# Gated net's spatial and output weights: loaded whole over their own low parts and split within the token mixer's last batch

## What is computed

```python
# 1: gated linear attention, 8 heads of 48, state over t
state = f[:, :, t, :, None] * state + einsum('bhd,bhe->bhde', k[:, :, t], v[:, :, t])
y[:, :, t] = einsum('bhd,bhde->bhe', q[:, :, t], state)
# 2: token mixer
theta = x @ w_theta
zr, zi = x * cos(theta), x * sin(theta)
u = x + einsum('ts,bsd->btd', w_tok_r, zr) + einsum('ts,bsd->btd', w_tok_i, zi)
x2 = u + maximum(u @ w_ch, 0)
# 3: gated net, d_ff = 1024, halves of 512
h = maximum(x2 @ w_in, 0);  u, v = halves of h
v_n = (v - mean(v)) / sqrt(var(v) + 1e-6)
v_s = einsum('ts,bsd->btd', w_spatial, v_n) + b_spatial
out = (u * v_s) @ w_out
```

## Time and profile before

| | us |
|---|---|
| Median of 3 runs | 621.71 (621.22 to 622.42) |
| The profiled execution, its own time | 619.17 |
| Its span, first to last instruction | 617.2 |
| PE busy | 580.9 (94%) |
| DVE busy | 367.0 (59%) |
| ACT busy | 290.6 (47%) |
| POOL busy | 34.7 (6%) |
| Share of DMA queue q1 in 16 engines' span | 31.4% |

### The profile page before, as it was taken

The page is one execution under the profiler, slowest core; times in us unless marked ns, Lnnn a source line. Parts: engine busy times, 40 slices in busy tenths (PEclk is TensorE's granted clock), DMA queues, the critical chain, the costliest instruction groups (busy, mean ns, idle before and its releaser), DMA issues.

```text
span 617.2 us, 11905 instructions
## 1 busy us (share of the span) xinstructions
PE 580.9 (94%) x4226; PEld 559.9 (91%) x4226; DVE 367.0 (59%) x614; ACT 290.6 (47%) x509; POOL 34.7 (6%) x66
## 2 busy tenths in 40 slices
PE   0999998789999999999999999899999999999998
PEld 0888887689999999999999998898999899989997
DVE  7899998466776538454955557557145713571151
ACT  5799996765553335242644225415331533153112
POOL 3232332000000000000000000000000000000000
PEclk9999999879999999999999999899999999999999
DMA  7879999262410231022013243500040001000102
GB/s 187 201 228 246 267 252 314 59 219 93 192 38 27 65 102 39 25 76 89 0 43 115 76 144 109 207 2 1 25 129 2 0 25 51 0 1 27 52 0 78
DMA packets 31546, 58.76 MB, mean 95 GB/s; under 512 B 3728, under 2 KB 23184, under 8 KB 31504
## 3 DMA queue, kind: packets, MB, share of 16 engines
q1 hardware_dynamic: 31504, 58.21, 31.4%
HBM read 44.04 MB, written 14.16 MB: 94 GB/s over the span
## 4 chain that ended last, share of the span: by engine, by line
PE 72%; DVE 3%; issue 3%; ACT 1%; DMA 1%; DVEq 0%; ACTq 0%; SPq 0%
PE mix_ps L1054 24%; PE gate_ps L1054 16%; PE ringc L1054 10%; PE theta_bank L1054 10%; PE small_ps L1054 10%; PE small_ps L1436 1%; DVE stats L1998 1%; DVE w_lo L78 1%; DMA wc_stage<-in_wC_dram 1%; ACT w_hi L73 0%; ACT v L1848 0%; DVE vn L2016 0%; DVE ang L1574 0%; DVE ang L1571 0%; DVE z L1590 0%
## 5 line engine op out<-in xcount | busy, mean ns | idle before, releaser
L1054 PE MATMUL mix_ps<-w_lo,z_hi 128*128 128x384 f32 x288 | 97.3, 338 | 2.0 <-issue 2.0
L1054 PE MATMUL mix_ps<-w_hi,z_hi 128*128 128x384 f32 x288 | 99.0, 344 | 0.0
L1054 PE MATMUL mix_ps<-w_hi,z_lo 128*128 128x384 f32 x288 | 97.6, 339 | 0.0
L1054 PE MATMUL gate_ps<-w_hi 128*128 128x384 f32 x192 | 64.9, 338 | 4.1 <-issue 4.1
L1054 PE MATMUL gate_ps<-w_hi,w_lo 128*128 128x384 f32 x192 | 64.7, 337 | 0.0
L1054 PE MATMUL gate_ps<-w_lo,w_hi 128*128 128x384 f32 x192 | 64.7, 337 | 0.0
L1054 PEld LDWEIGHTS mix_ps<-w_hi,z_lo 128*128 128x128 f32 x288 | 54.6, 190 | 2.2 <-issue 2.2
L1054 PEld LDWEIGHTS mix_ps<-w_lo,z_hi 128*128 128x128 f32 x288 | 54.6, 190 | 0.0
L1054 PEld LDWEIGHTS mix_ps<-w_hi,z_hi 128*128 128x128 f32 x288 | 54.6, 189 | 0.0
L73 ACT ACTIVATE g_hi<-gate 128x384 fp32r<-128x384 f32 x32 | 16.8, 526 | 78.6 <-DVE gate L2048 78.6
L2044 DVE TENSOR_TENSOR gate<-gate_ps,b_all 128x384 f32<-128x384 f32 x32 | 17.8, 557 | 59.7 <-PE gate_ps L1054 59.5
(11 more groups left out here) (163 smaller groups left out, 1417.1 us busy)
## 6 DMA issues: line engine op xcount, KB each, us to landing
f_raw<-in_fT_dram SPq DMA_DIRECT2D x32, 144.0 KB, 3.9
k_raw<-in_kT_dram SPq DMA_DIRECT2D x32, 144.0 KB, 3.3
q_raw<-in_qT_dram SPq DMA_DIRECT2D x32, 144.0 KB, 3.8
v_raw<-in_vC_dram SPq DMA_DIRECT2D x16, 288.0 KB, 4.0
xT<-y_sb SPq DMA_DIRECT2D x32, 144.0 KB, 3.7
xt<-xT SPq DMA_DIRECT2D x8, 576.0 KB, 4.0
w_raw<-in_wB_dram SPq DMA_DIRECT2D x6, 768.0 KB, 6.7
u<-xT SPq DMA_DIRECT2D x8, 576.0 KB, 5.0
```

The costliest lines, as they stand in the source:

```text
L1054: done = pe.matmul(out, a, b, start=(first and n == 0), stop=(last and n == len(terms) - 1))
```

## The change

`wc_stage` and the staged loads are taken out. `SpatialWeights` holds the new semaphores. SP's `load_w_c` issues, in the mixer's round 4 and for batch 3, three loads of 2048 columns (1 MB each) from wC into the first 6144 columns of `w_raw`, that is, into the place of the low parts; it waits until PE has used the token weights of s = 0 to 3 of the last batch (`mix_used` at 4). ACT's `w_c_up(0)` to `(5)` stand in round 5 behind `u_up(1)`. DVE's `w_c_down(0)` to `(3)` stand between the additions of round 5, and the low parts 4 and 5 are split in the gated net at the two places where parts 0 and 1 were (`w_down(4)`, `w_down(5)`); the four later splits of DVE and all of ACT's are gone from the gated net. PE's program is the same.

```diff
--- before
+++ after
+WC_LOADS = 3
...
+class SpatialWeights:
+    def __init__(self, nc, ctx, w_hi, w_lo, w_raw):
+        self.w_hi, self.w_lo, self.w_raw = w_hi, w_lo, w_raw
+        self.raw_in = [ctx.enter_context(nc.semaphore(f"c_raw_in{i}")) for i in range(WC_LOADS)]
+        self.hi_done = ctx.enter_context(nc.semaphore("c_whi_done"))
+        self.lo_done = ctx.enter_context(nc.semaphore("c_wlo_done"))
+
+    def up(self, act, n):
+        cols = slice(n * PART, (n + 1) * PART)
+        act.wait_ge(self.raw_in[n * WC_LOADS // WC_PARTS], 16)
+        split_hi(act, self.w_hi[:, cols], self.w_raw[:, cols]).then_inc(self.hi_done, 1)
+
+    def down(self, dve, n):
+        cols = slice(n * PART, (n + 1) * PART)
+        dve.wait_ge(self.hi_done, n + 1)
+        split_lo(dve, self.w_lo[:, cols], self.w_raw[:, cols], self.w_hi[:, cols]).then_inc(self.lo_done, 1)
+
+    def wait_for(self, eng, cols):
+        eng.wait_ge(self.hi_done, -(-cols // PART))
+        eng.wait_ge(self.lo_done, -(-cols // PART))
...
@@ token_mix, sync
+            def load_w_c(b):
+                if last_batch(b):
+                    sp.wait_ge(mix_used.h, mix_used.at(b, 4))
+                    for i in range(WC_LOADS):
+                        at, n = i * WC_COLS // WC_LOADS, WC_COLS // WC_LOADS
+                        sp.dma_start(part(w_raw, at, n), part(wC, W_IN_COLS + at, n)).then_inc(spatial.raw_in[i], 16)
...
-                        + [(load_residual, 1), (load_w_in, 1)], 2, 1)
+                        + [(load_residual, 1), (load_w_in, 1), (load_w_c, 1)], 2, 1)
...
@@ token_mix, scalar
+            def w_c_up(n):
+                def f(b):
+                    if last_batch(b):
+                        spatial.up(act, n)
+                return f
...
-                    (z_up(1), 1), (to_turns(2), 1), (u_up(0), 2), (u_up(1), 2), (trigs(2), 1), (xn_out(3), 1), (weights_up(2), 1), (w_in_up(0), 1),
+                    (z_up(1), 1), (to_turns(2), 1), (u_up(0), 2), (u_up(1), 2)] + [(w_c_up(n), 2) for n in range(WC_PARTS)] + [(trigs(2), 1), (xn_out(3), 1), (weights_up(2), 1), (w_in_up(0), 1),
...
@@ token_mix, vector (w_c_down(n) calls spatial.down(dve, n) for the last batch)
-                    (z_down(2), 1), (reduce(3), 1), (add_channel(0), 2), (multiply(3), 1), (add_channel(1), 2),
+                    (z_down(2), 1), (reduce(3), 1), (add_channel(0), 2), (multiply(3), 1), (add_channel(1), 2), (w_c_down(0), 2),
...
@@ gated_net, sync
-            for n in range(WC_PARTS):
-                if n >= STAGES:
-                    sp.wait_ge(whi_done, n - STAGES + 1)
-                    sp.wait_ge(wlo_done, n - STAGES + 1)
-                sp.dma_start(stage[n % STAGES][:, :], part(wC, W_IN_COLS + n * PART, PART)).then_inc(w_in[n % STAGES], 16)
...
@@ gated_net, scalar
-            def w_up(n):
-                def f(b):
-                    if first(b):
-                        act.wait_ge(w_in[n % STAGES], 16 * (n // STAGES + 1))
-                        split_hi(act, part(w_hi, n * PART, PART), stage[n % STAGES][:, :]).then_inc(whi_done, 1)
-                return f
...
@@ gated_net, vector
-                        dve.wait_ge(whi_done, n + 1)
-                        split_lo(dve, part(w_lo, n * PART, PART), stage[n % STAGES][:, :], part(w_hi, n * PART, PART))\
-                            .then_inc(wlo_done, 1)
+                        spatial_weights.down(dve, n)
...
-                (moments(2), 1), (normalise(1), 1), (vn_down(0), 1), (w_down(0), 1),
+                (moments(2), 1), (normalise(1), 1), (vn_down(0), 1), (w_down(4), 1),
...
-                (moments(4), 1), (normalise(3), 1), (vn_down(2), 1), (w_down(1), 1),
+                (moments(4), 1), (normalise(3), 1), (vn_down(2), 1), (w_down(5), 1),
...
-                (w_down(2), 1), (w_down(3), 1), (w_down(4), 1), (x_lo, 0), (w_down(5), 1), (gates, 1)], 2)
+                (x_lo, 0), (gates, 1)], 2)
```

More of the change, by code:

```diff
@@ L1090, in v_group, with token_mix @@
             both(in_hi, in_lo, k * DFF + FH, FH)) for k in range(DT)]).then_inc(gates.v_ps.h, 1)
-def token_mix(nc, sems, gates, waits_passed, w_hi, w_lo, w_raw, wb_hi, wb_lo, wB, wC, in_hi, in_lo, in_raw, xt, xt_hi, xt_lo,
+class SpatialWeights:
[15 more added lines that the diff above has]
+        eng.wait_ge(self.lo_done, -(-cols // PART))
+def token_mix(nc, sems, gates, spatial, waits_passed, w_hi, w_lo, w_raw, wb_hi, wb_lo, wB, wC, in_hi, in_lo, in_raw, xt, xt_hi, xt_lo,
               xn, mixing, rest, ident, half_pi, xT, x2T):
@@ L1660, in add_channel, with w_c_down, f @@
                 return f
+            def w_c_down(n):
+                def f(b):
+                    if last_batch(b):
+                        spatial.down(dve, n)
+                return f
             def first_x():
@@ L1711, in token_mix, with gated_net @@
                 "const_ready": const_ready, "x2_done": x2_done, "x2_out": x2_out}
-def gated_net(nc, sems, block, gates, mixer, waits_passed, w_hi, w_lo, in_hi, in_lo, xt, xt_hi, xt_lo, eps, early, late, stage, wC, bias,
+def gated_net(nc, sems, block, gates, spatial_weights, mixer, waits_passed, w_hi, w_lo, in_hi, in_lo, xt, xt_hi, xt_lo, eps, early, late, bias,
               x2T, out):
@@ L1785, in weights_ready @@
             if first(b):
-                eng.wait_ge(whi_done, -(-cols // PART))
-                eng.wait_ge(wlo_done, -(-cols // PART))
+                spatial_weights.wait_for(eng, cols)
         @block.sync
@@ L2114, in attention_and_mixers @@
         tail_lo = Region(nc, w_lo_at + 4 * EARLY_COLS)
-        STAGE_AT = VN_AT + ST * FH
-        stage = [t for at in (w_hi_at, w_lo_at) for t in Region(nc, at + 4 * STAGE_AT).take(f"wc_stage{at}_", [128, PART])]
         flag_ready = sems.enter_context(nc.semaphore("flag_ready"))
@@ L2122, in attention_and_mixers @@
         theta_in = sems.enter_context(nc.semaphore("theta_in"))
+        spatial = SpatialWeights(nc, sems, w_hi, w_lo, w_raw)
         with ExitStack() as banks:
             gates = Gates(nc, sems, [banks.enter_context(nc.psum_tensor(name, [128, 512], F32)) for name in ("theta_bank", "small_ps")])
-            mixer = token_mix(nc, sems, gates, waits_passed, w_hi, w_lo, w_raw, wb_hi, wb_lo, wB, wC, in_hi, in_lo, in_raw,
+            mixer = token_mix(nc, sems, gates, spatial, waits_passed, w_hi, w_lo, w_raw, wb_hi, wb_lo, wB, wC, in_hi, in_lo, in_raw,
                               xt, xt_hi, xt_lo, xn, mixing, rest, ident, half_pi, x_by_batch, x2T)
@@ L2153, in attention_and_mixers @@
                 banks.enter_context(nc.psum_tensor(f"mixer_bank{_}", [128, 512], F32))
-            gated_net(nc, sems, block, gates, mixer, waits_passed, w_hi, w_lo, in_hi, in_lo, xt, xt_hi, xt_lo, eps, early, late, stage,
-                      wC, bias, x2T, out)
+            gated_net(nc, sems, block, gates, spatial, mixer, waits_passed, w_hi, w_lo, in_hi, in_lo, xt, xt_hi, xt_lo, eps, early, late,
+                      bias, x2T, out)
 _INS = ["qT", "kT", "fT", "vC", "wB", "wC", "bias"]
```

18 lines of the change are left out of this document (7 added, 11 removed).

## The result

| | before | after |
|---|---|---|
| Median, us | 621.47 (620.64 to 622.42, 4 runs) | 613.91 (613.55 to 615.63, 4 runs) |
| Profiled execution, own time, us | 619.17 | 613.82 |
| Its span, us | 617.2 | 611.9 |
| PE busy, us | 580.9 | 578.6 |

The ratio is 0.9883 (95% interval 0.986 to 0.9907): the change gains 7.3 us, between 5.8 and 8.7 us. The direction was right. The forecast started from the three runs known then (621.71 us); the table has a fourth. The two profiled executions, on which each step can be checked, are only 5.3 us apart.

A forecast was written before the change was run, and what follows sets the result against it. TensorE (PE) is busy nearly throughout, so gains come from its few stops, chiefly the wait for spatial weights. 4.22 + 1.45 + 0.25 - 0.2 = 5.7 us off 621.71 us gives 616.0 us, range 614.9 to 617.9 us.

The forecast's parts named there:

- The chain and the gap: PE ahead of batch 0's first spatial product: the wait for staged spatial weights goes, 4.22 us gained.
- The clock: Nine products behind that gap run at full clock instead of 1.2 GHz: 1.45 us gained.
- The second stop: PE's wait for ut at 381.11 us goes, without ACT's weight part ahead of vn's high part: 0.25 us gained.
- DVE's slip: Four splits between the mixer's last additions delay DVE by 0.2 us (0.84 us without overlap), all reaching PE.
- The first stop: PE's wait for ut at 379.26 us stays, since DVE still splits weights in the vn chain.
- ACT, SP, the transfers: ACT's six splits (5.8 us) and SP's three early loads (390 GB/s) fit into cover and cost nothing.
- The sum against the median: The 5.7 us summed on one profiled execution was taken off the runs' median, 621.71 us, giving 616.0 us.
- (a): Rival: DVE's additions in the mixer's last batch slip by 2 us; 617.8 us, chance 0.08.
- (b): Rival: weights land late, x2T stores are caught behind them, vn chain 7.4 us late; 623.2 us, chance 0.05.
- (c): Rival: an engine stops for instruction fetch behind the loads' backlog; up to 622.9 us, chance 0.03.
- (d): Rival: something other than the weights released the first spatial product, so the wait stays; chance 0.02.

The follow-up runs named there:

- The loads alone: The changed kernel with its three early loads kept but all ACT and DVE splits back in the gated net; median 614.99 us, ratio 0.9905 to before.
- filling the gap: The kernel before plus 22 unread products between batch 0's u products and the first spatial product; median 619.0 us, ratio 0.9972 to before.
- the second comparison: The changed kernel run again with no edit, against the kernel before; median 613.9 us, ratio 0.9899.
- late loads: The changed kernel with its three weight loads issued only after ACT's u splits, just ahead of the first x2T store; median 618.82 us, ratio 0.9967 to before.

## Why the prediction was right or wrong

**The chain and the gap: right.** What stood behind the gap was the staged load. The gap fell from 4.39 to 0.18 us, 4.21 us against 4.22 us forecast. The loads alone remove most of it.

**The clock: the mechanism right, the size wrong.** The step was "3.01 - 1.56 = 1.45 us go with the idle time that caused them". It took the length of the slow stretch from the one execution in the trace. In that execution it was right (1.49 - 0.02 us). But the stretch has two lengths, and three of five executions paid 2.6 us; the mean is 2.15 us, and filling the gap gained 1.7 us (0.8 to 2.7 us). The term should have been 2.13 us (2.15 - 0.02), 0.7 us more, with a range up to 2.6 us. This is the largest part of the miss that lies in the sum.

**The second stop: right.** 0.25 us forecast, 29.04 - 28.75 = 0.29 us measured. The first stop stayed, as forecast.

**DVE's slip: the size right, the conclusion wrong.** The additions slipped by 0.12 us without a wait (0.2 forecast), and by 0.4 to 0.6 us where the first store took longer to land (2.80 us in the third, 2.99 us in the first profile). But "all of it reaches PE" was wrong: nothing of it did, since DVE's queue releases v ahead of DVE: the moments came 8.92 to 8.94 us behind the first addition in all three, 8.92 us before. The step left out the 0.6 us between DVE's last addition and the first moments. That is 0.2 us of the error.

**ACT, SP, the transfers: right.** Cost nothing; the splits ran without idle time, and the loads came at 414 to 443 GB/s.

**The sum against the median: wrong.** "The terms are the same for either, so I forecast 621.71 - 5.7" set the sum of one execution on the median of the others. That execution was fast for two reasons: the short slow stretch, which is a term of the change itself, and an early start of the last batch (355.13 us; the five executions of before have a mean of 356.61 us), which is not. The corrected sum is 4.21 + 2.13 + 0.29 = 6.6 us, or by the traces 259.59 - 252.88 = 6.7 us (means of five and of three). From 621.47 us this gives 614.8 us. The interval of the ratio, 5.8 to 8.7 us, holds it; for the second comparison it is 5.0 to 7.6 us.

**What of the 2.1 us is the sum's, and what is scatter.** The clock's term was 0.7 us too small, DVE's 0.2 us too large, and the fourth run lowered the median of before by 0.2 us. With these the forecast would have been about 614.8 us, at the lower end of the range (614.9 us). The rest of 0.9 us looks like the scatter of few runs. All executions on record, 67 of before and 10 of the changed kernel, have means of 620.91 and 613.96 us. They are 6.9 us apart, some 0.8 us either way, where the traces give 6.7 us. The first medians were 7.6 us apart, and the traced executions of the changed kernel had the easy start told above (first addition at 354.90 us in the mean, clock 0.91). Why the clock of that stretch differs between executions stays open.

**The rivals.** (a) was not seen beyond 0.6 us and cost nothing. (b) didn't occur, but the experiment with late loads shows that stores behind such loads land late and hold the additions. (c) could not show in the changed kernel: its three traces have no instruction transfer while the loads were in flight (340 to 352 us in the first). With the late loads one did fall among them, on queue q8 at 355.9 us. Queue q8 and the busy times from 350 to 362 us of that run:

```profile
q8 instruction: 1, 0.02, 0.5%
```

```profile
350.00:362.00 12.00, 12.00 (x67) 11.40 (x66) 4.10 (x6) 5.00 (x6) 0.00 (x0) 1.00 0.80 296
```

PE was busy for all of the 12 us, so this one transfer, whose engine the trace doesn't name, cost it nothing. (d) is refuted.

## What to carry to other kernels

When idle time goes, count what the clock pays behind it over several executions, and don't subtract a sum made on one execution from a median of others before asking which of its stretches vary. Where an addition waits for a store on the same queue as big loads, issue the loads early enough to be in before the first store: 12 us earlier or later was worth 4.2 us here. A split moved out of a chain between two engines is worth more than one moved out of idle time: look for the place where PE still stops (here the two splits left in the vn chain, 0.58 us).

## What the runs showed that I had not expected

The slow stretch behind the same gap lasts 8 or 15 to 16 slow steps (1.4 to 1.5 us or 2.6 us lost), from execution to execution. After a shorter idle time, 2.19 us, the clock went down only when PE had been busy again for 1.3 us, and stayed down for 3.5 us. An engine's queue can release another engine's work ahead of its own: v on ACT started 0.97 us before the DVE addition that stands ahead of it in DVE's program.

And the first store of the last batch, 192 KB with no load or other store in flight, took 3.0 us to land in the first trace of the changed kernel and held DVE for 0.4 us, 2.8 us in the third, 1.9 us in the second. It happens in the kernel before too. There the third addition of the fifth execution waited for it, and the fourth was back in time, since DVE had 1 us to spare in each slot:

```profile
361.20 0.56 DVE L1658 SCALAR_TENSOR_TENSOR x<-mix_ps,u 128x384 f32<-128x384 f32 x1 [1.56 <-DMA x2T<-x]
```

What goes with it is a transfer of 16 KB on the instruction queue. From 356.4 to 359.4 us, the flight of the slow store in the first trace of the changed kernel:

```profile
q8 instruction: 1, 0.02, 3.0%
```

Leaving out the late loads, thirteen traces have this store. In five of them the instruction transfer started 0.3 to 0.7 us behind the store's issue, and the store took 2.5 to 3.0 us. In the other eight it started 1.1 to 1.4 us ahead of the issue, and the store took 1.86 to 1.87 us. No experiment moved the transfer, so that it is the cause isn't shown.
